# Second feed-forward stage with plain float32 matmuls over the whole array, and its inner layer on four 32-row strips

## The chip, the cores and the metric

One NeuronCore of a Trainium2 chip runs the whole kernel. TensorE multiplies, VectorE and ScalarE work on tiles in SBUF and read PSUM, GpSimd prepares some tiles in the first part, and the DMA queue that SyncE (SP) fills moves nearly all data. The metric is the device time of one execution in microseconds; the number to forecast is the median over the runs of the changed kernel.

## What is computed

A linear attention with decay (4 batches, 8 heads, 768 steps, heads of 48) gives x, 3072 tokens by 384. A soft mixture of 8 experts with 4 slots each follows, and then a feed-forward layer with a squared relu:

```
x = attention(r, k, v, w, u)                 # 3072 x 384
logits = x @ phi                             # 3072 x 32
d = softmax over tokens;  slot_input = d.T @ x          # 32 x 384
slot_out[e] = relu(slot_input[e] @ w1[e]) @ w2[e]       # 32 x 384
c = softmax over slots;   y = c @ slot_out   # 3072 x 384
h = relu(y @ w_in)                           # 3072 x 2048
out = (h * h) @ w_out                        # 3072 x 384
```

The last two lines are the second feed-forward stage, which the change is about.

## The kernel before

The kernel is written out per engine, with semaphores between them. Its first part (to about 360 us) is the attention, in eight rounds of loops over pairs of heads. Then come the transposes of x (L561), the logits (L584), the two softmaxes, the slots (L606), the experts' up projection (L624, in four 32-column strips of the array) and down projection (L647, `down`), and the transposes of c into `c_st` (L668, copied out by `copy_ct`).

The second stage never forms y. Since y @ w_in = c @ (slot_out @ w_in), the kernel first makes m = slot_out @ w_in, 32 x 2048. L680 writes it into one PSUM bank: row strip q of 32 partitions holds columns 512q to 512q + 511. So the inner layer is a contraction over 32 slots.

Before the change this stage runs on split operands. `F32R` (fp32r) is a data type of reduced precision for matmul operands; the trace has one record for such a matmul. A float32 tile is taken apart into a high part, rounded to F32R, and a low part, the rest. For m and c the parts lie one above the other on the 128 partitions: `c_rep` has four copies of c per token block, high, high, low, low (L873 and L1165), and `m_parts`, `spread` and L690 lay m out as `m_st`, 128 x 2048, so that one matmul over 128 rows adds the four cross products. For the outer layer `wo_high` and `wo_low` hold w_out in parts, made from `w_raw` in four quarters by ScalarE (`wo_split_high`, L295) and VectorE (`wo_split_low`, L1180).

The loop goes over 8 groups of three token blocks (384 tokens) and in each over 16 blocks fb of 128 inner features, 128 steps in all:

- TensorE, `hidden` (L698): one matmul, 384 tokens wide, two steps ahead, into one of two banks.
- ScalarE, `hidden_sq`: relu (L907), then square (L911).
- VectorE, `split`: `h_high` is the rounded copy (L1210), `h_low` the rest (L1212).
- TensorE, `product`: for each of the three token blocks high x high, high x low, low x high (L708, L709, L710) into that block's accumulator bank. Two sets of three accumulator banks alternate.
- ScalarE, `out_copy` (L918), in the second step of the next group: three accumulators into `o_sb`; SP stores them (L372).

SP starts w_out's transfers after the last transpose of c (L365), two quarters, and the other two as `w_raw` comes free (L368). The order of the work on each engine is the order of the code.

Of the kernel before, what the change touches and what calls it, by code (L numbers as in the profile page):

```python
# [22 lines left out]
F32 = mybir.dt.float32  # L23
# [7 lines left out]
def fused_kernel(nc, r, k, v, w, u, phi, w1, w2, w_in, w_out, out, debug=None):  # L31
# [23 lines left out]
    with ctx:  # L55
# [6 lines left out]
        def sem2(name):  # L62
# [11 lines left out]
        c_stack = ExitStack()  # L74

        c_rep = sb("c_rep", [P, NT, 4, SL], F32R, c=c_stack)
        c_stack.close()
        w_raw = sb("w_raw", [P, 2, 4, E_DIM])
# [41 lines left out]
        wo_high = sb("wo_high", [P, NF, E_DIM], F32R, c=over_w1)  # L120
        wo_low = sb("wo_low", [P, NF, E_DIM], F32R, c=over_w1)
# [9 lines left out]
        c_st = sb("c_st", [P, B * S], F32R, c=fin)  # L131
        m_st = sb("m_st", [P, DFF], F32R, c=fin)
        h_relu = [sb(f"h_relu{i}", [P, GT * P], c=fin) for i in range(2)]
        h_sq = [sb(f"h_sq{i}", [P, GT * P], c=fin) for i in range(2)]
        h_high = [sb(f"h_high{i}", [P, GT * P], F32R, c=fin) for i in range(2)]
        h_low = [sb(f"h_low{i}", [P, GT * P], F32R, c=fin) for i in range(2)]
# [12 lines left out]
        h_stack = ExitStack()  # L149
        h_sb = sb("h_sb", [P, FF], c=h_stack)  # L150
        h_stack.close()
        m_parts = sb("m_parts", [P, 2, 512], F32R)
        h_t = sb("h_t", [P, 2, FB, P])
        small = sb("small", [P, 256])
        spread = sb("spread", [P, 2, 4, SL], F32R)
# [47 lines left out]
        w_raw_loaded = [sem(f"w_raw_loaded{i}") for i in range(2)]  # L203
# [10 lines left out]
        m_full, m_high, m_low, m_rep = sem("m_full"), sem("m_high"), sem("m_low"), sem("m_rep")  # L214
        m_rep_copy = [sem(f"m_rep_copy_{e}") for e in ("act", "dve")]
        spread_set, c_high, c_low, ct_full = sem("spread_set"), sem("c_high"), sem("c_low"), sem("ct_full")
        ct_copy = [sem(f"ct_copy_{e}") for e in ("act", "dve")]
        wo_high_done, wo_low_done = sem("wo_high_done"), sem("wo_low_done")
        h_mm, relu_done, sq_done, high_done, low_done = (sem(n) for n in ("h_mm", "relu_done", "sq_done", "high_done",
                                                                          "low_done"))  # L220
        prod_mm, o_copy = sem("prod_mm"), sem("o_copy")
# [9 lines left out]
        acc_bank = (bank[0:3], bank[3:6])  # L231
        h_bank = bank[6:8]
        M_BANKS = (0, 3, 4, 5)
        WO_SPLIT_AT = (1, 4, 8)
# [57 lines left out]

        def wo_split_high(act, part):
            act.wait_ge(w_raw_loaded[part % 2], 16 * (part // 2 + 1))
            nc.scalar.activation(wo_high[:, 4 * part:4 * part + 4, :], w_raw[:, part % 2], ACT.Copy)\  # L295
                .then_inc(wo_high_done, 1)

        @block.sync
        def _(sp):
# [66 lines left out]
            for i in range(2):  # L366
                sp.wait_ge(wo_low_done, i + 1)
                sp.dma_start(w_raw[:, i], wo_v[:, 4 * (i + 2):4 * (i + 2) + 4]).then_inc(w_raw_loaded[i], 16)  # L368

            def store(g, par):  # L370
                sp.wait_ge(o_copy, GT * (g + 1))
                sp.dma_start(out_v[bass.ds(GT * g, GT)].rearrange("n p d -> p n d"), o_sb[par][:])\  # L372
                    .then_inc(stored[par], 16)

            with sp.Fori(0, GROUPS // 2) as gg:
                for par in range(2):
                    store(gg * 2 + par, par)
            for par in range(2):
                sp.wait_ge(stored[par], 16 * GROUPS // 2)

# [872 lines left out]
```

## Time and profile before

| | us |
|---|---|
| median of 3 runs | 645.51 |
| lowest, highest of these runs | 641.88, 651.84 |
| span of the profiled execution | 648.8 |
| busy in that span: TensorE, weight loads, VectorE, ScalarE, GpSimd | 519.0, 445.8, 436.0, 397.5, 64.7 |
| mean granted TensorE clock | 0.908 |

The profiled execution's own time is not given apart from these runs; its span of 648.8 us, from the first to the last instruction, lies between the second and the third of them. A granted clock of 1.00 is 2.4 GHz, 0.50 is 1.2 GHz. "PE" is TensorE's matmuls and "PEld" its weight loads; a matmul's record lasts until its last result is written, so records of matmuls that follow one another overlap. "w_hi", "w_lo" and "w_sb" are names that the profile gives to w2_hi, w2_lo and w1_sb.

### The profile page before, as it was taken

The numbers are of one execution on the slowest core, as the hardware profiler recorded it, in microseconds if no ns is written. First come the engines' busy times: TensorE is split into PE (matmuls) and PEld (weight loads), VectorE is DVE, ScalarE is ACT, GpSimd is POOL, SyncE is SP. The second block draws the span as 40 slices with busy tenths as digits, with TensorE's granted clock in tenths as the row PEclk, the third lists the DMA queues.
The fourth block names the chain that finished last, engine by engine and source line by source line (L and its number), as shares of the span: only waits on it lengthen the run. The fifth ranks groups of instructions, "written<-read, shape, count | busy, mean of one in ns | idle before, by whom it ended". The sixth has DMA issues, their size and how long they took to land.

```text
span 648.8 us, 20419 instructions
## 1 busy us (share of the span) xinstructions
PE 519.0 (80%) x8010; PEld 445.8 (69%) x8010; DVE 436.0 (67%) x968; ACT 397.5 (61%) x753; POOL 64.7 (10%) x79
## 2 busy tenths in 40 slices
PE   3756766877668668766686798699999999999996
PEld 2544655756457447564576434399999999999996
DVE  5668999898688688896797441465555555555553
ACT  3648686885576477865765313466566666656563
POOL 4011213112031031130310000000000000000000
PEclk9869898987698699886887899899999999999999
DMA  9995354362154143630057699311010101101010
GB/s 140 303 314 98 62 96 68 73 109 54 24 109 78 30 83 76 108 60 17 3 113 257 225 387 364 141 52 37 2 37 1 38 1 36 37 0 36 1 37 36
DMA packets 143325, 60.75 MB, mean 94 GB/s; under 512 B 126496, under 2 KB 139808, under 8 KB 142880
## 3 DMA queue, kind: packets, MB, share of 16 engines
q1 hardware_dynamic: 141264, 51.97, 33.9%
q10 hardware_dynamic: 2000, 7.86, 3.2%
q8 instruction: 51, 0.84, 0.6%
q14 instruction: 10, 0.08, 0.0%
HBM read 55.10 MB, written 4.72 MB: 92 GB/s over the span
## 4 chain that ended last, share of the span: by engine, by line
PE 63%; issue 13%; DVE 11%; ACT 10%; ACTq 1%; DVEq 1%; DMA 0%; SPq 0%
PE bank L708 11%; PE bank L710 10%; PE bank L709 10%; PE lbank L497 7%; ACT rkw L756 6%; PE tbank L449 4%; PE ybank L523 4%; PE bank L698 3%; DVE wprod L992 3%; DVE a_pack L1046 2%; PE tbank L459 2%; DVE rkw L1012 2%; PE bank L647 2%; PE bank L624 2%; PE bank L561 1%
## 5 line engine op out<-in xcount | busy, mean ns | idle before, releaser
L708 PE MATMUL bank<-wo_high,h_high 128*128 128x384 f32 x384 | 129.6, 337 | 1.8 <-DVE h_low L1212 1.6
L709 PE MATMUL bank<-wo_low,h_high 128*128 128x384 f32 x384 | 128.9, 336 | 0.0
L710 PE MATMUL bank<-wo_high,h_low 128*128 128x384 f32 x384 | 128.9, 336 | 0.0
L497 PE MATMUL lbank<-rhat,rkw 128*32 128x64 f32 x3456 | 81.5, 244 | 53.9 <-DVE a_pack L1046 36.8
L791 ACT ACTIVATE rhat<-rkw 48x384 f32<-48x384 f32 x160 | 85.0, 531 | 59.5 <-PE lbank L497 42.2
L497 PEld LDWEIGHTS lbank<-rhat,rkw 128*32 128x32 f32 x3456 | 69.9, 126 | 63.7 <-issue 61.9
L1210 DVE CAST h_high<-h_sq 128x384 fp32r<-128x384 f32 x128 | 46.0, 360 | 96.7 <-PE bank L710 87.9
L907 ACT ACTIVATE h_relu<-bank 128x384 f32<-128x384 f32 x128 | 62.9, 492 | 74.4 <-PE bank L698 74.1
L756 ACT ACTIVATE rkw<-tbank 128x384 f32<-128x384 f32 x96 | 74.4, 876 | 20.5 <-PE tbank L449 20.5
L449 PE MATMUL tbank<-ident,nat 128*128 128x128 f32 x288 | 62.7, 358 | 29.7 <-ACT rkw L756 16.7
L708 PEld LDWEIGHTS bank<-wo_high,h_high 128*128 128x128 f32 x384 | 72.6, 189 | 3.2 <-issue 2.8
L1212 DVE TENSOR_TENSOR h_low<-h_sq,h_high 128x384 fp32r<-128x384 f32 x128 | 71.5, 559 | 4.4
L449 PEld LDWEIGHTS tbank<-ident,nat 128*128 128x128 f32 x288 | 39.4, 175 | 50.7 <-ACT rkw L756 35.2
L709 PEld LDWEIGHTS bank<-wo_low,h_high 128*128 128x128 f32 x384 | 72.7, 189 | 0.0
L710 PEld LDWEIGHTS bank<-wo_high,h_low 128*128 128x128 f32 x384 | 72.5, 189 | 0.0
L911 ACT ACTIVATE h_sq<-h_relu 128x384 f32<-128x384 f32 x128 | 67.4, 527 | 4.1
L1012 DVE TENSOR_TENSOR rkw<-rkw,wprod 128x384 f32<-128x384 f32 x80 | 45.4, 571 | 15.3 <-PE lbank L497 14.8
L408 POOL COPY mov<-state 48x576 f32<-48x576 f32 x28 | 35.2, 1258 | 170.9 <-DVE state L1054 170.1
L1046 DVE COPY_PREDICATED a_pack<-masks,lbank 128x384 f32<-128x384 int32 x80 | 46.5, 581 | 0.2
L1001 DVE TENSOR_TENSOR rkw<-rkw,wprod 128x384 f32<-128x384 f32 x64 | 41.1, 642 | 5.0 <-ACT rhat L791 4.1
L698 PE MATMUL bank<-c_st,m_st 128*128 (+1 forms) x126 | 42.7, 339 | 0.3 <-ACT h_relu L907 0.3
L976 DVE COPY rhat<-rkw 48x384 f32<-48x384 f32 x32 | 16.5, 515 | 29.0 <-ACT rkw L756 28.4
(129 smaller groups left out, 639.2 us busy)
## 6 DMA issues: line engine op xcount, KB each, us to landing
w_sb<-in_moe_w_dram ACTq DMA_DIRECT2D x5, 1536.0 KB, 15.7
w_hi<-in_moe_w_dram SPq DMA_DIRECT2D x16, 384.0 KB, 8.1
nat<-in_r_dram SPq DMA_DIRECT2D x32, 144.0 KB, 3.2
nat<-in_k_dram SPq DMA_DIRECT2D x32, 144.0 KB, 3.8
nat<-in_w_dram SPq DMA_DIRECT2D x32, 144.0 KB, 3.9
mov<-in_v_dram SPq DMA_DIRECT2D x32, 144.0 KB, 3.3
v_tok<-in_v_dram SPq DMA_DIRECT2D x32, 144.0 KB, 3.3
w_sb<-in_moe_w_dram SPq DMA_DIRECT2D x3, 1536.0 KB, 7.4
```

What stands on the lines that cost most here:

```text
L449: last = nc.tensor.transpose(bank[:, i * P:(i + 1) * P], src, ident[:])
L497: last = nc.tensor.matmul(dst.rearrange("p (h t) -> p h t", h=2), kk[:, t0:t0 + SUB], rhat[s][:, :, tt:tt + SUB], start=True, stop=True)
L698: nc.tensor.matmul(h_bank[fb % 2][:, 0:GT * P], m_st[:, fb * P:(fb + 1) * P], c_st[:, bass.ds(g * (GT * P), GT * P)], start=True, stop=Tru ...
L708: nc.tensor.matmul(acc, hi, wo_high[:, fb, :], start=(fb == 0), stop=False)
L709: nc.tensor.matmul(acc, hi, wo_low[:, fb, :], start=False, stop=False)
L710: last = nc.tensor.matmul(acc, lo, wo_high[:, fb, :], start=False, stop=(fb == NF - 1))
L756: nc.scalar.activation(dst, src, ACT.Copy).then_inc(t_evac, 1)
L791: nc.scalar.activation(half_split(rhat[s][a:b, h, :], 1 << lv)[:, :, 1, :], half_split(rkw[s][a:b, 0, :], 1 << lv)[:, :, 1, :], ACT.Copy)\
L907: nc.scalar.activation(h_relu[fb % 2][:], h_bank[fb % 2][:, 0:GT * P], ACT.Relu).then_inc(relu_done, 1)
L911: nc.scalar.activation(h_sq[fb % 2][:], h_relu[fb % 2][:], ACT.Square).then_inc(sq_done, 1)
L1046: nc.vector.copy_predicated(a_pack[s][:].rearrange("p c h t -> p (c h) t"), mask, data)\
L1212: nc.vector.tensor_tensor(h_low[i][:], h_sq[i][:], h_high[i][:].bitcast(F32), ALU.subtract)\
```

## The change

The stage drops the split. `wo_sb` holds w_out as it is, `m_sb` is one copy of the PSUM bank with m, in its four row strips (128 x 512), and `c_rep` is four plain copies of c. The 128 blocks of the inner layer become 32 steps of four: step n is group g = n // 4 and k = n % 4, and its strip r (32 rows) gives feature block 4r + k. `hidden(n)` issues four matmuls over 32 rows each, into four banks. ScalarE does only the relu, VectorE multiplies the result by itself, into eight tiles. `product(n, r)` is three plain float32 matmuls of 128 rows, one per token block. The accumulators rotate through four banks, and at a group's start only the second and third matmul wait for an output copy. SP loads w_out in one transfer as soon as w1's place is free, behind the transfers of w2_hi, and the last group is stored block by block. The loops are written out.

The core of the diff:

```diff
-        wo_high = sb("wo_high", [P, NF, E_DIM], F32R, c=over_w1)
-        wo_low = sb("wo_low", [P, NF, E_DIM], F32R, c=over_w1)
+        wo_sb = sb("wo_sb", [P, NF, E_DIM], c=over_w1)
...
-        acc_bank = (bank[0:3], bank[3:6])
-        h_bank = bank[6:8]
+        h_bank = (bank[0], bank[1], bank[6], bank[7])
+        acc_bank = (bank[3], bank[4], bank[5], bank[2])
+        KS = NF // 4
+        STEPS = GROUPS * KS
+
+        def acc_of(n):
+            return acc_bank[n % 4]
...
-            sp.wait_ge(ct_full, CT_USES)
-            for i in range(2):
-                sp.dma_start(w_raw[:, i], wo_v[:, 4 * i:4 * i + 4]).then_inc(w_raw_loaded[i], 16)
...
+            sp.wait_ge(up_mm, 4)
+            sp.dma_start(wo_sb[:], wo_v).then_inc(wo_loaded, 16)
...
+            def hidden(n):
+
+                g, k = divmod(n, KS)
+                cols = slice(g * GT * P, (g + 1) * GT * P)
+                for r in range(4):
+                    if n:
+                        pe.wait_ge(relu_done, 4 * (n - 1) + r + 1)
+                    rows = slice(SL * r, SL * r + SL)
+                    nc.tensor.matmul(h_bank[r][:, 0:GT * P], m_sb[rows, k * P:(k + 1) * P], c_st[rows, cols],
+                                     start=True, stop=True).then_inc(h_mm, 1)
+
+            def product(n, r):
+                g, k = divmod(n, KS)
+                pe.wait_ge(sq_done, 4 * n + r + 1)
+                first, final = k == 0 and r == 0, k == KS - 1 and r == 3
                 for i in range(GT):
...
+                    at = GT * g + i
+                    if first and at >= 4:
+                        pe.wait_ge(o_copy, at - 3)
+                    last = nc.tensor.matmul(acc_of(at)[:, 0:E_DIM], h_sq[4 * (n % 2) + r][:, i * P:(i + 1) * P],
+                                            wo_sb[:, KS * r + k, :], start=first, stop=final)
+                    if i < GT - 1 and final:
+                        last.then_inc(acc_done, 1)
                 last.then_inc(prod_mm, 1)
...
+            pe.wait_ge(m_copied, 1)
+            hidden(0)
+            pe.wait_ge(wo_loaded, 16)
+            for n in range(STEPS):
+                for r in range(4):
+                    if r == 2 and n + 1 < STEPS:
+                        hidden(n + 1)
+                    product(n, r)
...
+            nc.scalar.activation(m_sb[:], bank[2][:, :], ACT.Copy).then_inc(m_copied, 1)
...
+            for n in range(STEPS):
+                g, k = divmod(n, KS)
+                for r in range(4):
+                    act.wait_ge(h_mm, 4 * n + r + 1)
+                    if n:
+                        act.wait_ge(sq_done, 4 * (n - 1) + r + 1)
+                    nc.scalar.activation(h_relu[r][:], h_bank[r][:, 0:GT * P], ACT.Relu).then_inc(relu_done, 1)
+                if k == 0 and g:
+                    for i in range(GT):
+                        out_copy(GT * (g - 1) + i)
...
             for q in range(2):
-                nc.vector.tensor_tensor(c_part(2 + q), cc[:], c_part(q).bitcast(F32), ALU.subtract).then_inc(c_low, 1)
...
+                nc.vector.tensor_copy(c_part(2 + q), cc[:]).then_inc(c_spread, 1)
...
+            for n in range(STEPS):
+                for r in range(4):
+                    dve.wait_ge(relu_done, 4 * n + r + 1)
+                    if n >= 2:
+                        dve.wait_ge(prod_mm, 4 * (n - 2) + r + 1)
+                    nc.vector.tensor_tensor(h_sq[4 * (n % 2) + r][:], h_relu[r][:], h_relu[r][:], ALU.mult)\
+                        .then_inc(sq_done, 1)
```

On TensorE, from m (L680) to the first products, the order before is:

```order
L680 MATMUL bank<-w_in_sb,slot_ot 32x512 x11
L690 MATMUL bank<-m_parts,spread 128x512 [waits m_low,m_high,spread_set]
L690 MATMUL bank<-m_parts,spread 128x512 x7
L730 MATMUL bank<-c_st,m_st 128x384 [waits m_rep_copy_act]
L730 MATMUL bank<-c_st,m_st 128x384
L698 MATMUL bank<-c_st,m_st 128x384 [waits relu_done]
L708 MATMUL bank<-wo_high,h_high 128x384 [waits low_done,high_done,wo_low_done]
L709 MATMUL bank<-wo_low,h_high 128x384
L710 MATMUL bank<-wo_high,h_low 128x384
```

and now, where L659, L671 and L682 are the lines of m, `hidden` and `product`:

```order
L659 MATMUL bank<-w_in_sb,slot_ot 32x512 x11
L671 MATMUL bank<-c_st,m_sb 128x384 [waits m_copied]
L671 MATMUL bank<-c_st,m_sb 128x384 x3
L682 MATMUL bank<-wo_sb,h_sq 128x384 [waits sq_done,wo_loaded]
L682 MATMUL bank<-wo_sb,h_sq 128x384 x2
L682 MATMUL bank<-wo_sb,h_sq 128x384 [waits sq_done]
L682 MATMUL bank<-wo_sb,h_sq 128x384 x2
L671 MATMUL bank<-c_st,m_sb 128x384 [waits relu_done] x4
```

The eight matmuls that lay m out are gone, one block of the inner layer per nine products has become four strips per twelve, and the first product waits for the load of all of w_out.

On TensorE at the start of the third group now, with its waits:

```order
L671 MATMUL bank<-c_st,m_sb 128x384 [waits relu_done] x4
L682 MATMUL bank<-wo_sb,h_sq 128x384 [waits sq_done]
L682 MATMUL bank<-wo_sb,h_sq 128x384 x2
L682 MATMUL bank<-wo_sb,h_sq 128x384 [waits sq_done]
L682 MATMUL bank<-wo_sb,h_sq 128x384 x2
L682 MATMUL bank<-wo_sb,h_sq 128x384 [waits sq_done]
L682 MATMUL bank<-wo_sb,h_sq 128x384 [waits o_copy] x2
```

The next step's strips stand two product blocks ahead of its first product, and of a group's first three matmuls the second and third wait for a copy.

## Rows read from the trace of the kernel before

**Rows 1.** the page's chain that ended last, by line

```profile
PE bank L708 11%; PE bank L710 10%; PE bank L709 10%; PE lbank L497 7%; ACT rkw L756 6%; PE tbank L449 4%; PE ybank L523 4%; PE bank L698 3%; DVE wprod L992 3%; DVE a_pack L1046 2%; PE tbank L459 2%; DVE rkw L1012 2%; PE bank L647 2%; PE bank L624 2%; PE bank L561 1%
```

**Rows 2.** stretches by busy us (instructions) of each engine, clock, DMA share, GB/s

```profile
413.40:419.61 6.21, 2.23 (x12) 0.96 (x12) 4.62 (x7) 5.84 (x9) 0.00 (x0) 0.75 0.06 11
419.61:643.96 224.35, 224.15 (x1277) 222.82 (x1277) 121.19 (x257) 138.54 (x276) 0.00 (x0) 0.99 0.07 26
643.96:648.80 4.84, 0.00 (x0) 0.00 (x0) 0.00 (x0) 1.25 (x3) 0.00 (x0) 0.98 0.33 122
453.28:481.04 27.76, 27.76 (x161) 27.75 (x161) 14.70 (x32) 17.34 (x35) 0.00 (x0) 1.00 0.06 23
416.60:423.40 6.80, 4.92 (x15) 4.11 (x14) 5.76 (x9) 4.49 (x9) 0.00 (x0) 0.50 0.42 121
```

**Rows 3.** one group by lines: count, busy us, mean ns, idle before

```profile
L710 PE MATMUL bank<-wo_high,h_low 128*128 128x384 f32 x48 | 16.0, 334 | 0.0
...
L1212 DVE TENSOR_TENSOR h_low<-h_sq,h_high 128x384 fp32r<-128x384 f32 x16 | 8.9, 559 | 0.6
...
L907 ACT ACTIVATE h_relu<-bank 128x384 f32<-128x384 f32 x16 | 7.9, 492 | 9.4 <-PE bank L698 9.4
```

**Rows 4.** line L602, its weight loads in time, and that stretch

```profile
L602 PE MATMUL bank<-dd,ones x4: 844/844/1006, 370.3 to 372.4; 128*128 128x384 f32 x4
...
371.10 0.33 PEld L602 LDWEIGHTS bank<-dd,ones 128*128 128x128 f32 x1 [0.30 <-issue]
371.74 0.33 PEld L602 LDWEIGHTS bank<-dd,ones 128*128 128x128 f32 x1 [0.31 <-issue]
...
370.40:373.20 2.80, 2.80 (x8) 1.11 (x11) 1.24 (x3) 0.84 (x1) 0.00 (x0) 0.50 1.07 376
```

**Rows 5.** in order of time after m, and line L690 (durations ns min/median/max)

```profile
413.40 0.60 ACT L895 ACTIVATE m_parts<-bank 128x512 fp32r<-128x512 f32 x1 [3.88 <-PE bank L680]
...
414.87 0.75 PE L690 MATMUL bank<-m_parts,spread 32*128 32x512 f32 x8 [1.53 <-DVE m_parts L1196]
...
L690 PE MATMUL bank<-m_parts,spread x8: 391/427/496, 414.9 to 415.2; 32*128 32x512 f32 x8
```

**Rows 6.** float32 on four column strips, L647

```profile
403.59 5.37 PE L647 MATMUL bank<-w_hi,h_t 128*32 128x384 f32 x64
...
L647 PE MATMUL bank<-w_hi,h_t x64: 486/486/510, 403.6 to 408.5; 128*32 128x384 f32 x64
```

**Rows 7.** column strips, whole array, strips again, in time; lines and clock

```profile
272.30 0.68 PE L497 MATMUL lbank<-rhat,ku 128*32 128x64 f32 x35
272.90 1.60 PE L505 MATMUL ybank<-ones 128*128 128x128 f32 x12
274.44 0.77 PE L497 MATMUL lbank<-rhat,rkw 128*32 128x64 f32 x40
...
272.90 0.71 PE L505 MATMUL ybank<-ones 128*128 128x128 f32 x4
...
L505 PE MATMUL ybank<-ones x160: 275/275/582, 22.6 to 339.0; 128*128 128x128 f32 x160
...
L497 PE MATMUL lbank<-rhat,rkw x3456: 216/219/316, 27.0 to 338.0; 128*32 128x64 f32 x192
...
272.50:275.00 2.50, 2.50 (x87) 2.29 (x79) 2.47 (x7) 2.40 (x5) 0.00 (x0) 1.00 1.20 185
```

**Rows 8.** the DMA engines ahead of the products

```profile
404.00:410.00 6.00, 5.39 (x67) 2.07 (x59) 0.39 (x1) 0.49 (x1) 0.00 (x0) 1.00 0.98 334
410.00:416.00 6.00, 3.65 (x34) 1.02 (x32) 1.39 (x5) 2.37 (x3) 0.00 (x0) 1.00 0.01 2
```

**Rows 9.** VectorE's relu h_sb, behind c_low and spread, and line L624

```profile
386.78 0.68 DVE L1174 TENSOR_SCALAR h_sb<-bank 128x512 f32<-128x512 f32 x1
...
L624 PE MATMUL bank<-w_sb,slot_t x96: 592/592/617, 380.3 to 390.2; 128*32 128x512 f32 x96
```

**Rows 10.** the last output copies, after the last product

```profile
643.99 1.25 ACT L918 ACTIVATE o_sb<-bank 128x384 f32<-128x384 f32 x3 [3.63 <-PE bank L710]
```

More of the change, by code:

```diff
@@ L130, in fused_kernel @@
         fin = ExitStack()
[L131 to L136, printed above, removed]
+        c_st = sb("c_st", [P, B * S], c=fin)
+        m_sb = sb("m_sb", [P, DFF // 4], c=fin)
+        h_relu = [sb(f"h_relu{i}", [P, GT * P], c=fin) for i in range(4)]
+        h_sq = [sb(f"h_sq{i}", [P, GT * P], c=fin) for i in range(8)]
         o_sb = [sb(f"o_sb{i}", [P, GT, E_DIM], c=fin) for i in range(2)]
@@ L213, in fused_kernel @@
         down_mm, so_copy, so_turned, so_ready = sem("down_mm"), sem("so_copy"), sem("so_turned"), sem("so_ready")
[L214 to L216 removed]
+        m_full, m_copied = sem("m_full"), sem("m_copied")
+        c_spread, ct_full = sem("c_spread"), sem("ct_full")
         ct_copy = [sem(f"ct_copy_{e}") for e in ("act", "dve")]
[L218 to L221, printed above, removed]
+        h_mm, relu_done, sq_done = sem("h_mm"), sem("relu_done"), sem("sq_done")
+        prod_mm, acc_done, o_copy = sem("prod_mm"), sem("acc_done"), sem("o_copy")
         stored = [sem("stored0"), sem("stored1")]
@@ L660, in _ @@
             turn_slots(0)
-            pe.wait_ge(c_high, 2)
-            pe.wait_ge(c_low, 2)
+            pe.wait_ge(c_spread, 4)
             for n in range(CT_USES):
@@ L682, in _ @@
             last.then_inc(m_full, 1)
-            pe.wait_ge(spread_set, 8)
-            pe.wait_ge(m_high, 1)
-            pe.wait_ge(m_low, 1)
-            for n in range(4):
-                rows = slice(SL * n, SL * n + SL)
-                for x in range(2):
-                    last = nc.tensor.matmul(bank[M_BANKS[n]][:, :], spread[rows, x].rearrange("p q j -> p (q j)"),
-                                            m_parts[rows, x, :], start=(x == 0), stop=(x == 1))
-                last.then_inc(m_rep, 1)
@@ L713, in group @@
-            def group(g, par, lead=True, wait_acc=True, first=False):
-                for fb in range(NF):
-                    if fb < NF - 2:
-                        if first and fb % 4 == 2:
-                            n = (fb + 2) // 4
-                            pe.wait_ge(m_rep_copy[n % 2], n // 2 + 1)
-                        hidden(g, fb + 2)
-                    elif lead:
-                        hidden(g + 1, fb + 2 - NF)
-                    if fb == 0 and wait_acc:
-                        pe.wait_ge(o_copy, GT * (g - 1))
-                    if first and fb % 4 == 0:
-                        pe.wait_ge(wo_low_done, fb // 4 + 1)
-                    product(g, par, fb)
@@ L728, in _ @@
-            pe.wait_ge(m_rep_copy[0], 1)
-            for fb in range(2):
-                nc.tensor.matmul(h_bank[fb][:, 0:GT * P], m_st[:, fb * P:(fb + 1) * P], c_st[:, 0:GT * P],
-                                 start=True, stop=True).then_inc(h_mm, 1)
-            group(0, 0, wait_acc=False, first=True)
-            group(1, 1, wait_acc=False)
-            with pe.Fori(1, GROUPS // 2 - 1) as gg:
-                group(gg * 2, 0)
-                group(gg * 2 + 1, 1)
-            group(GROUPS - 2, 0)
@@ L913, in out_copy @@
-            def out_copy(g, par, first=False):
-                act.wait_ge(prod_mm, NF * (g + 1))
-                if not first:
-                    act.wait_ge(stored[par], (g - par) * 8)
-                for i in range(GT):
-                    nc.scalar.activation(o_sb[par][:, i, :], acc_bank[par][i][:, 0:E_DIM], ACT.Copy)\
-                        .then_inc(o_copy, 1)
-            def group(g, par, before=True, first=False):
-                for fb in range(NF):
-                    hidden_sq(g, fb, fresh=(not before and fb < 2))
-                    if not before and fb in WO_SPLIT_AT:
-                        wo_split_high(act, WO_SPLIT_AT.index(fb) + 1)
-                    if fb == 1 and before:
-                        out_copy(g - 1, 1 - par, first)
```

134 lines of the change are left out of this document (27 added, 107 removed).

## The prediction

> **What bounds the kernel now.** I read the chain that ended last first. It puts 63% of the span on TensorE, and its three largest lines are the three products of the second feed-forward stage, L708 to L710 [rows 1]. Then the stretches by stage [rows 2]: that stage runs from 419.61 to 643.96 us, 224.35 us or 35% of the span, and TensorE is busy for 224.15 of it. Then one group of it by lines [rows 3]: 144 product records and 16 hidden-layer records fill 27.76 us, so 0.1735 us from one matmul to the next. A record lasts 0.334 us, about twice that, because each overlaps its neighbour: it is the spacing that counts, not the duration. VectorE is busy for 14.70 and ScalarE for 17.34 of the 27.76 us. So this stage is bound by TensorE's columns, and what matters is how many passes of 384 columns the changed stage makes and at what spacing.
>
> All my sums are made inside the profiled execution, whose span is 648.8 us. The runs shown are 641.88, 645.51 and 651.84 us; only the last is long enough to contain that span, with 3.0 us around it. I work out a difference of spans and add it to the median, 645.5. About 2% (13 us) is what a measurement of this kernel can tell from no change.
>
> **The change part by part.**
>
> *Products, the large term.* Removed: 1152 split products of 384 columns at 0.1735 us, 199.9 us. Added: 384 matmuls (32 steps of 4 strips of 3 blocks) in plain float32. What does one cost? The kernel has plain float32 matmuls already. L602 issues two, of 128x128 against 384 columns, exactly the shape of the new ones, and the trace has four records [rows 4]: one such matmul is two records. They run while the granted clock is 0.50 (1.2 GHz), and the weight loads of the last two start 0.64 us apart (371.10, 371.74). At 2.4 GHz that is 0.32 us for a record, two cycles per column, where a split matmul at that clock takes 0.1735 for one record of as many columns. There are two such records to a matmul, so a block costs four passes of 384 columns where it cost three.
> At the high clock there is a small addition to each record. Bounds: in four column strips L647 puts 64 records into 5.37 us [rows 6]; less the last one's 0.486 that is 4.88 over 15 steps of four, 0.325 each. No addition at all, 0.320, is the lowest. The split products have 0.0135 over the ideal 0.160; the same on each 0.320 gives 0.3335, the highest. The row nearest in shape is L505, a plain float32 128x128 matmul of 128 columns at the clock of 1.00: 12 records in 1.60 us, 4 in 0.71 [rows 7], so 8 spacings in 0.89, 0.111 each, where 0.32 us for 384 columns would be 0.107 for 128. That is 0.004 to 0.005 on top, weight load of 128 columns included. Both point to 0.325, and I take that. 384 x 2 x 0.325 = **249.6 us** (245.8 to 256.1). A weight load under each record is no term of its own: L505 hides one under 0.111 us.
>
> *Hidden layer on four strips.* Removed: 128 matmuls at 0.1735, 22.2 us (two of them before 419.61). Added: 32 rounds of four 32-row matmuls, 31 of them inside the stage. In m_rep's matmuls (L690) the kernel has four row strips of 32: eight records of 512 columns lie within 0.75 us [rows 5], where one after the other they would need 8 x 512/384 x 0.16 = 1.7 us. So strips do overlap, even though the two matmuls of a strip stand next to each other in the program. Two float32 records per strip are then 0.645 us for all four. In L690 the last record, of 0.39 us, starts 0.75 - 0.39 = 0.36 us after the first, 0.15 more than 512 columns take (0.213): I add 0.15. Crossing between strips and the whole array also costs: the last L497 record starts at 272.98 - 0.22 = 272.76, L505 at 272.90; that is 0.14 where fours of L497 follow each other at (0.68 - 0.22) / 8.5 = 0.055, 0.09 more. L505's first spacing is 0.71 - 0.275 - 2 x 0.111 = 0.21, 0.10 more than its others. Back, L497 starts at 274.44, 0.21 after the last L505 (272.90 + 1.60 - 0.275 = 274.23), again 0.10 more [rows 7]. Together 0.29 per round trip. So a round is 0.645 + 0.15 + 0.29 = 1.08 us and 31 of them **33.5 us**. Bounds: 0.65 (no crossing, no stagger), 20.2 us; or strips that don't overlap at all, which is a rival below.
> By the Trainium skill, TensorEngine Tiling (Array Packing), section Key Properties, changing the tiling mode drains the TensorE. The trace shows less than that: by its recorded ends L505 begins 0.08 us before L497 is over. If each of the 62 crossings waited for the recorded end (0.486 - 0.325 = 0.16 us, [rows 6], instead of some 0.095), the sum would be 4 us higher, 706 us.
>
> *Clock.* After the idle stretch ahead of the products, TensorE stood at 1.2 GHz from 416.6 to 423.4 us [rows 2], 3.8 us of it under products: 1.9 us lost. The new start has idle waits of the same kind, so I keep **1.9 us** (0 to 3.4).
>
> *The stage.* 249.6 + 33.5 + 1.9 + 0.2 for the last record's tail = 285.2 against 224.35.
>
> *Start.* Now: m_full, split into m_parts, spread (L690), m_st, first hidden block, relu, square, and on VectorE a wo_low ahead of m_st's second part and h_high: 413.40 to 419.61, 6.21 us [rows 2]. New: one copy of m (0.60, as that of m_parts, [rows 5]), strips from 414.03, first strip done after 0.15 + 0.32 + 0.49 = 0.96 at 415.0, relu 0.49, multiply 0.56 (h_low's subtraction, two operands of the same size, [rows 3]), some 0.05 of waiting: first product at 416.1. **Minus 3.5 us.** It also needs the whole w_out. SP now issues it in one transfer right behind the 16 of w2_hi, not in quarters from 403.7 on. The DMA engines are full until 410 (0.98 busy, 334 GB/s) and then idle (2 GB/s) [rows 8], and half of w_out (1.57 MB) is already in that traffic. The other half takes 1.57 MB at 334 GB/s = 4.7 us: it lands near 414.7. Hidden, with 1.4 us to spare; if all of it came after 410, products would start at 419.4, 3.3 us later. It has nothing behind it on SP until the first store. The work taken from VectorE and ScalarE earlier (c_low, spread, the wait of c_low for c_high) ends when VectorE turns to h_sb at 386.78, and TensorE needs that only behind L624, whose last record starts at 390.2 [rows 9]: nothing gained.
>
> *Per step beside TensorE.* A step is 24 x 0.325 + 1.08 = 8.9 us. ScalarE has four relus (2.0 us), VectorE four multiplies (2.2 us). Behind the strips of the next step stand two product blocks of 3 x 0.65 = 1.95 us each, 3.9 us, and the first multiply is due 1.1 us after its strip. The wait for an output copy at a group's start covers itself: the freed block was finished three matmuls (1.95 us) earlier, the copy takes 0.49. Both hidden; uncovered they would cost 7 to 8 group starts x 0.5 = 4 us.
>
> *End.* Three copies after the last product (1.25 us, [rows 10]) become one (0.49): **minus 0.8 us**. The last store is a third in size; I keep the 3.6 us behind the copies (bound: 1.2 us less).
>
> Sum: 416.1 + 285.2 = 701.3, + 4.84 - 0.76 = 705.4 us of span, 56.6 more than 648.8. 645.5 + 56.6 = **702.1 us**, 8.8% slower.
>
> **The rivals.**
> A (other side): whole-array float32 records run at the pace of the split ones, 0.174 us, at the high clock. Then products are 768 x 0.174 = 133.6 us and the span 589, the time 586 us. It decides from 0.251 us per record (235.4 us from 413.40 to the end, less 42.4 of new fixed terms, over 768); with 0.268 it would be 2% slower. For: fewer instructions, and no row has this exact shape at 2.4 GHz. Against: L602 and L505 both show two cycles per column in every record.
> B: 32-row strips in float32 don't overlap. Each round is 4 x 0.65 + 0.44 = 3.04, 31 x 1.96 = 61 us more, 763 us. For: L690 is split, not float32. Against: L690 overlaps with its pair of matmuls per strip, L647 overlaps in float32 on column strips.
> C: weight loads for float32 are laid bare, 0.10 us a record (what L505's first spacing shows over its others): 77 us more, 779 us. Against: L505's later spacings, L602's 0.64.
> D: the products start late or wait once per group (w_out, copies): 2 to 6 us, inside my range.
>
> **How the numbers follow.** Forecast 0.90, A 0.03, B 0.04, C 0.03. The forecast's own range: low, 20.2 instead of 33.5 for the strips and 3.8 less in records, 685; high, 6.5 more for the products and 3.3 for w_out, 712. Both extremes at once are unlikely, but the runs before spread by some 4 to 6 us either way: 688 to 717. That holds about 8 in 10 with the rivals left out. Faster by over 2%: only A, 0.02. Within 2%: A in part, 0.01. Slower by over 2%: 0.97.
>
> **What would show it.** Right: two records per product matmul, weight loads hidden, spacing 0.325; the stage some 285 us long; steps of 8.9 us, of which the strips take about 1.1; first product near 416; VectorE and ScalarE under a third busy there, clock 1.00. Wrong: record spacing below 0.27 (A) or above 0.4 (C), rounds of strips near 3 us (B), product matmuls that wait for sq_done or o_copy, a first product after 418.

## The result, and the profile after

The changed kernel takes 704.43 us (median of 4 runs, 697.38 to 705.90) against 646.83 us for the kernel before (4 runs, 641.88 to 651.84): a ratio of 1.088 with a 95% interval of 1.080 to 1.096. It is slower by nearly 9%, and the forecast was 702.1 us. All ratios leave out runs that were over 1.5% above the fastest of the same kernel. The profiled execution has a span of 704.0 us, 55.2 more than before; I had worked out 56.6.

The page's table of engines, the lines of the new stage and its clock answer to [rows 1, 3]:

```profile
PE 581.1 (83%) x7746; PEld 382.1 (54%) x7746; DVE 370.7 (53%) x825; ACT 317.6 (45%) x619; POOL 65.3 (9%) x79
...
PEclk9989978669985799868889999999999999999999
...
L682 PE MATMUL bank<-wo_sb,h_sq 128*128 128x384 f32 x768 | 256.2, 490 | 1.2 <-DVE h_sq L1127 1.2
L682 PEld LDWEIGHTS bank<-wo_sb,h_sq 128*128 128x128 f32 x768 | 143.3, 190 | 112.0 <-issue 16.9
L1127 DVE TENSOR_TENSOR h_sq<-h_relu 128x384 f32<-128x384 f32 x128 | 62.9, 554 | 214.2 <-ACT h_relu L869 214.2
L869 ACT ACTIVATE h_relu<-bank 128x384 f32<-128x384 f32 x128 | 52.4, 496 | 199.7 <-PE bank L671 199.7
...
L671 PE MATMUL bank<-c_st,m_sb 32*128 32x384 f32 x256 | 29.7, 533 | 0.7 <-ACT m_sb L851 0.7
```

Each of the 384 product matmuls is two records (x768), each of the 128 strip matmuls too (x256). TensorE is all but never idle before them (1.2 us), while VectorE and ScalarE sit idle some 200 us: the stage is bound by TensorE alone, more so than before. The slices of the stage stand at clock 9, which means 90% or more.

By stretches, in the columns of [rows 2] (copy of m to first product; the loop; from the last product's end; one step of the loop):

```profile
417.66:420.48 2.82, 0.93 (x8) 0.34 (x9) 0.70 (x2) 1.82 (x5) 0.00 (x0) 1.00 0.22 78
420.48:701.10 280.62, 280.62 (x1016) 152.93 (x1016) 62.17 (x127) 62.50 (x149) 0.00 (x0) 1.00 0.04 15
701.10:704.00 2.90, 0.00 (x1) 0.00 (x0) 0.00 (x0) 0.49 (x1) 0.00 (x0) 1.00 0.57 203
566.10:574.89 8.79, 8.79 (x36) 4.79 (x32) 1.96 (x4) 1.64 (x4) 0.00 (x0) 1.00 0.01 2
```

Start 2.82 us (6.21 before), loop 280.62 (224.35), end 2.90 (4.84). From the copy of m to the end of the span that is 286.3 us instead of 235.4: 50.9 us of the 55.2 arise in the changed stage. The other 4.3 lie ahead of it: the copy of m starts at 417.66 instead of 413.40. There the code is the same but for the copies of c and the time at which w_out's load is issued, and its place in time varies between executions. In the profiles below, all of nearly the same code up to there, the copy starts at anything from 411.6 to 418.7. The new load isn't the cause of the shift: 3.9 of the 4.3 us were there at the first up projection (384.24 instead of 380.30), and the load is issued at 402.8.

One step of the loop on TensorE, and what ScalarE and VectorE do beside it:

```profile
566.10 8.01 PE L682 MATMUL bank<-wo_sb,h_sq 128*128 128x384 f32 x24
566.18 1.64 ACT L869 ACTIVATE h_relu<-bank 128x384 f32<-128x384 f32 x4 [4.22 <-PE bank L671]
566.71 1.96 DVE L1127 TENSOR_TENSOR h_sq<-h_relu 128x384 f32<-128x384 f32 x4 [6.83 <-ACT h_relu L869]
...
574.03 0.93 PE L671 MATMUL bank<-c_st,m_sb 32*128 32x384 f32 x8
...
574.89 1.56 PE L682 MATMUL bank<-wo_sb,h_sq 128*128 128x384 f32 x4
```

A column gives the start, the next the time to the end of the last record. 24 product records (12 matmuls: the last two blocks of one step and the first two of the next) begin at 566.10, the strips at 574.03, the next products at 574.89. A step is 574.89 - 566.10 = 8.79 us. The products' 24 records end at 574.11, and the last one lasts 0.486: so from the first start to the last it is 7.52 us, over 23 spacings. The first of these is 0.43 (1.56 us for four records at 574.89, less 0.486 and two spacings), the others 0.3225 each. VectorE's last multiply ends at 568.67, 2.6 us after the products start. The next step's first product is the 13th record, at about 570.1, so ScalarE and VectorE have at least 1.4 us to spare.

### The profile page after: what moved, and what is told of

Its sections match the earlier page's. It is cut to its first block, busy times and chain, and to the rows that moved or that the text cites. A ratio compares the mean times of both kernels' runs of the same rounds, so it can differ in the third digit from the quotient of the medians.

```text
span 704.0 us, 19073 instructions
## 1 busy us (share of the span) xinstructions
PE 581.1 (83%) x7746; PEld 382.1 (54%) x7746; DVE 370.7 (53%) x825; ACT 317.6 (45%) x619; POOL 65.3 (9%) x79
## 4 chain that ended last, share of the span: by engine, by line
PE 63%; issue 12%; ACT 10%; DVE 10%; SPq 2%; DMA 2%; ACTq 1%; DVEq 1%
PE bank L682 36%; PE lbank L477 6%; ACT rkw L713 6%; PE tbank L429 4%; PE bank L671 4%; PE ybank L503 4%; DVE wprod L930 2%; DVE a_pack L984 2%; PE lbank L453 2%; SPq L345 2%; DVE rkw L950 2%; PE tbank L439 1%; DMA w_hi<-in_moe_w_dram 1%; DVE rkw L939 1%; PE bank L541 1%
## 5 line engine op out<-in xcount | busy, mean ns | idle before, releaser
L682 PE MATMUL bank<-wo_sb,h_sq 128*128 128x384 f32 x768 | 256.2, 490 | 1.2 <-DVE h_sq L1127 1.2
L682 PEld LDWEIGHTS bank<-wo_sb,h_sq 128*128 128x128 f32 x768 | 143.3, 190 | 112.0 <-issue 16.9
L1127 DVE TENSOR_TENSOR h_sq<-h_relu 128x384 f32<-128x384 f32 x128 | 62.9, 554 | 214.2 <-ACT h_relu L869 214.2
L429 PEld LDWEIGHTS tbank<-ident,nat 128*128 128x128 f32 x288 | 40.2, 178 | 50.9 <-ACT rkw L713 35.0
L503 PE MATMUL ybank<-mov,stat 112*64 112x48 f32 (+1 forms) x768 | 32.1, 245 | 4.4 <-issue 4.4
L503 PEld LDWEIGHTS ybank<-mov,stat 112*64 112x64 f32 (+1 forms) x768 | 29.7, 158 | 7.1 <-issue 6.5
L398 POOL COPY stat<-rkw 48x384 f32<-48x384 f32 x32 | 23.0, 720 | 100.2 <-DVE rkw L939 97.3
L671 PE MATMUL bank<-c_st,m_sb 32*128 32x384 f32 x256 | 29.7, 533 | 0.7 <-ACT m_sb L851 0.7
L930 DVE TENSOR_TENSOR wprod<-wprod 128x192 f32<-128x192 f32 (+4 forms) x80 | 27.2, 340 | 0.0
L439 PE MATMUL tbank<-ident,rkw 112*128 112x112 f32 x96 | 16.7, 311 | 12.0 <-issue 9.3
L992 DVE TENSOR_TENSOR_SCAN state<-w_scan,kv 112x576 f32<-112x576 f32 x16 | 21.7, 1354 | 4.4 <-ACT kv L728 4.4
```

Of the source, the lines that this page charges most:

```text
L429: last = nc.tensor.transpose(bank[:, i * P:(i + 1) * P], src, ident[:])
L503: last = nc.tensor.matmul(ybank[C * par:C * par + C, o:o + D], stat[s][h][0:rows, c, :], mov[s][h][0:rows, c, :], start=True, stop=True)
L671: nc.tensor.matmul(h_bank[r][:, 0:GT * P], m_sb[rows, k * P:(k + 1) * P], c_st[rows, cols], start=True, stop=True).then_inc(h_mm, 1)
L682: last = nc.tensor.matmul(acc_of(at)[:, 0:E_DIM], h_sq[4 * (n % 2) + r][:, i * P:(i + 1) * P], wo_sb[:, KS * r + k, :], start=first, stop= ...
L1127: nc.vector.tensor_tensor(h_sq[4 * (n % 2) + r][:], h_relu[r][:], h_relu[r][:], ALU.mult)\
```

## The experiments

Since the unchanged part shifts by several microseconds from one execution to the next, I compare, next to the times, three stretches of each profile, cut as above: start, loop, end.

| kernel | start | loop | end | from copy of m | time, us |
|---|---|---|---|---|---|
| before | 6.21 | 224.35 | 4.84 | 235.4 | 646.8 |
| changed | 2.82 | 280.62 | 2.90 | 286.3 | 704.4 |
| plain products only | 4.73 | 271.86 | 4.93 | 281.5 | 695.0, ratio 1.069 (1.058 to 1.080) |
| strips only | 4.77 | 240.98 | 2.94 | 248.7 | 664.1, ratio 1.017 (1.005 to 1.029) |
| no rounds | 2.82 | 249.61 | 2.91 | 255.3 | 672.3 |
| double rounds | 3.46 | 300.62 | 2.91 | 307.0 | 722.6 |
| rounds cut in two | 2.82 | 314.20 | 2.86 | 319.9 | 740.4 |
| late load | 2.82 | 282.32 | 2.85 | 288.0 | 707.4 |
| bfloat16 parts | 6.21 | 214.49 | 4.85 | 225.6 | 643.2, ratio 0.984 (0.969 to 1.000) |
| combined | 5.29 | 212.18 | 3.03 | 220.5 | 639.8, ratio 0.981 (0.971 to 0.991) |

Ratios are to runs of the kernel before that were made beside each kernel. Their median was 652.1 us beside the plain products, the strips and the bfloat16 parts, and 652.7 us beside the combined kernel, not the 646.8 us of the result. Times are medians of all runs of a kernel; one without a ratio, from the third row on, is a single run. Each kernel has one profile.

**One part alone: plain float32 products.** The inner layer stays one split matmul per block.

```diff
                 for i in range(GT):
                     acc = acc_bank[par][i][:, 0:E_DIM]
-                    hi, lo = (a[fb % 2][:, i * P:(i + 1) * P] for a in (h_high, h_low))
-                    nc.tensor.matmul(acc, hi, wo_high[:, fb, :], start=(fb == 0), stop=False)
-                    nc.tensor.matmul(acc, hi, wo_low[:, fb, :], start=False, stop=False)
-                    last = nc.tensor.matmul(acc, lo, wo_high[:, fb, :], start=False, stop=(fb == NF - 1))
+                    last = nc.tensor.matmul(acc, h_sq[fb % 2][:, i * P:(i + 1) * P], wo_sb[:, fb, :],
+                                            start=(fb == 0), stop=(fb == NF - 1))
```

> The kernel before with only the outer layer changed to plain float32 products (w_out whole, in one transfer); the inner layer stays one split matmul over the whole array per block. Theory (a float32 record of 384 columns is 0.3225 us, a round of strips 1.055 us): the loop holds 768 x 0.3225 + 126 x 0.1735 = 269.6 us against 280.6 of the changed kernel, the start is some 1.7 us longer and the end 0.8 us, so 704.4 - 11.0 + 2.5 = 696 us. Rival (the strips are what made it slow, by waits or crossings that the sum put elsewhere): 670 us or less. Rival (changing between float32 and split matmuls costs like a crossing, 0.4 us per step of 128): 745 us.

Measured 695.0 us. The loop, and the pace in it:

```profile
411.58:416.31 4.73, 2.37 (x12) 1.12 (x12) 1.98 (x3) 2.84 (x6) 0.00 (x0) 0.81 0.06 23
416.31:688.17 271.86, 271.86 (x894) 168.46 (x893) 0.00 (x0) 122.44 (x275) 0.00 (x0) 0.99 0.04 16
```

```profile
560.01 2.10 PE L696 MATMUL bank<-wo_sb,h_sq 128*128 128x384 f32 x6
561.65 0.63 PE L688 MATMUL bank<-c_st,m_st 128*128 x1
562.12 2.10 PE L696 MATMUL bank<-wo_sb,h_sq 128*128 128x384 f32 x6
```

Steps stand 2.11 us apart (560.01, 562.12): six float32 records at 0.3225 and 0.17 for the split one between them, with no price for the change of type. 271.86 us of loop is 2.3 above the 269.6 expected. The clock explains that: a stretch at 1.2 GHz reached 5 us into the products (granted clock 0.51 from 416.31 to 421.40 us) and cost 2.5. The plain products alone bring 46.1 of the 50.9 us from the copy of m: they are the change's cost, and both rivals fall. That the time came within 1 us of the 696 expected is in part luck, since the kernel before was 5.3 us slower beside this run than in the result.

**The other part alone: strips.** The changed kernel with split products, their parts made by ScalarE and VectorE, and w_out loaded in four parts as before.

```diff
                 for i in range(GT):
...
-                    last = nc.tensor.matmul(acc_of(at)[:, 0:E_DIM], h_sq[4 * (n % 2) + r][:, i * P:(i + 1) * P],
-                                            wo_sb[:, KS * r + k, :], start=first, stop=final)
+                    acc = acc_of(at)[:, 0:E_DIM]
+                    hi, lo = (a[r][:, i * P:(i + 1) * P] for a in (h_high, h_low))
+                    nc.tensor.matmul(acc, hi, wo_high[:, 4 * k + r, :], start=first, stop=False)
+                    nc.tensor.matmul(acc, hi, wo_low[:, 4 * k + r, :], start=False, stop=False)
+                    last = nc.tensor.matmul(acc, lo, wo_high[:, 4 * k + r, :], start=False, stop=final)
```

> The changed kernel with only its inner layer kept (four row strips in plain float32, 32 steps), its products in split form as before, their parts made by VectorE and ScalarE. Theory: the loop is 1152 x 0.1735 + 31 x 1.055 = 232.6 us against 224.35 before, the start about 2 us shorter, the end 1 us, no time at the low clock 2 us: 646.8 + 3 = 650 us. Rival (strips save what they were meant to, 4 x 0.1735 become 0.65 with crossings hidden): 643 us. Rival (ScalarE's square and VectorE's split no longer keep up with four strips at once): above 660 us, with products waiting for low_done.

Measured 664.1 us, a miss: 14 us above the theory, ratio 1.017 where I had said 1.005. About 5 of the 14 us are in the kernel before too (652.1 instead of 646.8). The loop is 8.4 us longer than the 232.6 I gave it, and the waits in it (who waited for whom: us in total, times, longest) name one part:

```profile
417.41:422.18 4.77, 0.93 (x8) 0.34 (x9) 2.73 (x4) 4.67 (x9) 0.00 (x0) 0.86 0.00 0
422.18:663.16 240.98, 237.80 (x1400) 210.59 (x1400) 120.02 (x257) 129.82 (x277) 0.00 (x0) 0.99 0.07 25
```

```profile
PEld bank L698 <- ACT o_sb L886: 5.4, 7, 0.8
```

At seven group starts TensorE waits for the output copies, 0.77 us each, 5.4 in all. In the changed kernel it never does. The rows of the first such start here:

```profile
452.85 0.33 PE L700 MATMUL bank<-wo_high,h_low 128*128 128x384 f32 x1
...
454.24 0.52 ACT L896 ACTIVATE h_sq<-h_relu 128x384 f32<-128x384 f32 x1
454.67 1.24 ACT L886 ACTIVATE o_sb<-bank 128x384 f32<-128x384 f32 x3
...
455.20 0.44 PE L698 MATMUL bank<-wo_high,h_high 128*128 128x384 f32 x1 [0.45 <-ACT o_sb L886]
```

The group's first accumulator had its last record at 452.85, so it was complete at 453.2, but ScalarE began to copy it only at 454.67, right behind the last square. Four relus and four squares take it 3.8 us per step here, and the copies stand behind them in its order. In the changed kernel it has the relus alone (1.64 us), and there all 24 copies wait for a product. So the wait comes from ScalarE's squares and from where the copies stand. That is read from the trace; no run moved the copies. Another 2.7 us are the low clock at the start (granted clock 0.51 from 422.18 to 427.80 us). 5.4 + 2.7 = 8.1 of 8.4 us. The first rival falls (strips save nothing: a round is 1.06 us here too). The second is half right: no product waits for low_done in the loop, but ScalarE's squares do hold the products up, by way of the copies. The start was 4.77 us where I expected some 4.2: the first product waited for the first part of w_out's low half. From the copy of m to the end, the four kernels of this two by two give 46 us for the products, 13 for the strips, and 51, not 59, for both. Of these 8.5 us less, 5.4 are the copies' waits, which the changed kernel doesn't have, and 3.3 are the clock (1.9 us lost before, 2.5 with plain products, 2.7 with strips, none in the changed kernel).

**Rounds left out.** This kernel leaves the inner layer, relu and square out after the first step and multiplies the first four tiles again, so products no longer wait for squares.

```diff
                 for r in range(4):
-                    if r == 2 and n + 1 < STEPS:
-                        hidden(n + 1)
                     product(n, r)
```

> The changed kernel without the inner layer after the first step: products use the first four tiles again, so relu and squares are left out too. Theory: 31 rounds x 1.055 us go, and from the copy of m to the end it takes 286.3 - 32.7 = 253.6 us, with float32 records 0.3225 us apart throughout; the time is near 704 - 33 = 671 us. Rival (crossings cost nothing, a round is worth only its records, 0.65 us): 266 us from the copy, 684 in all. Rival (products also wait on relu or squares somewhere): below 248 us from the copy.

```profile
415.16:417.98 2.82, 0.93 (x9) 0.35 (x9) 0.71 (x2) 1.82 (x5) 0.00 (x0) 1.00 0.09 34
417.98:667.59 249.61, 249.61 (x768) 146.82 (x768) 1.25 (x3) 11.68 (x25) 0.00 (x0) 0.99 0.05 17
```

The span is 670.5 us. The loop of 249.61 us is 768 x 0.3225 = 247.7, the last record's 0.2 and 1.7 for 3.4 us at the low clock just behind the start (granted clock 0.54 from 417.98 to 421.70 us). Without that clock the rounds weigh 280.62 - 247.9 = 32.7 us, 31 x 1.055. The 1.055 was itself taken from the changed kernel's loop; what this run shows is that the 32.7 us go with the rounds, to 0.1 us, and that the first rival (0.65 us a round) and the second (products that wait) fall; 255.3 us from the copy of m lies 1.7 above the 253.6 expected, by the clock.

**Each round twice.**

```diff
-                for r in range(4):
-                    if n:
+                for x in range(2):
+                    for r in range(4):
+                        if n and not x:
...
+                        if x:
+                            last.then_inc(h_mm, 1)
```

> The changed kernel with each round of four strips issued twice, back to back, into the same banks. Theory (a round is 0.645 us of records and 0.41 us of crossing and bare weight loads, paid once per round trip): 32 x 0.645 = 20.6 us more, span 725 us. Rival (the 0.41 us belongs to every round of 128-column weights in 32-row strips): 32 x 1.055 = 33.8 us more, 738 us. Rival (strips of the second round overlap the first): less than 10 us more.

```profile
417.27:717.89 300.62, 300.62 (x1264) 165.72 (x1264) 62.17 (x127) 62.49 (x149) 0.00 (x0) 1.00 0.04 14
```

```profile
562.91 1.57 PE L672 MATMUL bank<-c_st,m_sb 32*128 32x384 f32 x16
564.41 8.01 PE L685 MATMUL bank<-wo_sb,h_sq 128*128 128x384 f32 x24
```

The loop grows by 300.62 - 280.62 = 20.0 us, 0.645 for each of its 31 rounds: 16 strip records in 1.57 us instead of 8 in 0.93. A second round costs its two records and nothing else. So 0.645 + 0.41 is the right split, the 0.41 us is paid per round trip, and both rivals fall.

**Each round cut in two.**

```diff
-                    if r == 2 and n + 1 < STEPS:
-                        hidden(n + 1)
+                    if r in (1, 2) and n + 1 < STEPS:
+                        hidden(n + 1, range(2 * r - 2, 2 * r))
```

> The changed kernel with each round of four strips cut in two: strips 0 and 1 after a step's first product block, strips 2 and 3 after its second. Same matmuls, twice the crossings, two strips side by side instead of four. Theory (a round costs 0.645 us of records and 0.41 us of crossing, whatever the number of strips in it): the loop grows by 31 x 1.055 = 32.7 us to 313 us, some 737 us in all. Rival (strips share the array's time, two cost half of four): 31 x 0.41 = 12.7 us more, 717 us. Rival (the crossing hides behind products when fewer strips wait): no change.

```profile
421.54:735.74 314.20, 314.20 (x1016) 159.79 (x1016) 64.97 (x127) 65.81 (x149) 0.00 (x0) 0.99 0.04 14
```

```profile
562.87 0.92 PE L671 MATMUL bank<-c_st,m_sb 32*128 32x384 f32 x4
563.71 2.20 PE L682 MATMUL bank<-wo_sb,h_sq 128*128 128x384 f32 x6
565.84 0.91 PE L671 MATMUL bank<-c_st,m_sb 32*128 32x384 f32 x4
```

The loop is 314.20 us. Less 1.7 for the clock that fell behind the start (0.62 from 421.54 to 426.00 us) it is 312.5, 31.9 more than the changed kernel's; 32.7 were expected. Two strips take as long as four (4 records in 0.91, 8 in 0.93), and each further round trip costs 0.4 us. Both rivals fall.

**The load of w_out late.**

```diff
-            sp.wait_ge(up_mm, 4)
+            sp.wait_ge(ct_full, CT_USES)
             sp.dma_start(wo_sb[:], wo_v).then_inc(wo_loaded, 16)
```

> The changed kernel with w_out's one transfer issued behind the last transpose of c, as before the change, instead of behind TensorE's last up projection. Theory (the DMA engines are full until it has landed, so they set the landing and not the time of issue, some 4 us later): start and total as in the changed kernel, 2.8 us from the copy of m to the first product, 286 us from that copy to the end. Rival (the early issue is what hides the load): first product 3 to 5 us later, 290 us from the copy. It also shows whether the experts' down projection then still waits for w2_hi (0.8 us in the changed kernel): by the theory it waits as long, since the queue works in order; by the rival that w_out's transfer takes bandwidth from w2_hi's, it does not.

In both kernels the rows are the issue by SP, the time to landing, and TensorE's longest wait for w2_hi (w_hi), first the changed kernel's:

```profile
402.83 0.95 SPq L348 DMA_DIRECT2D wo_sb<-in_moe_w_out_dram  x1
```

```profile
DMA to landing us min/median/max: 17.3/17.3/17.3
```

```profile
  PEld bank L627: 0.8, 1
```

and with the late load:

```profile
407.91 0.37 SPq L348 DMA_DIRECT2D wo_sb<-in_moe_w_out_dram  x1
```

```profile
DMA to landing us min/median/max: 11.9/11.9/11.9
```

```profile
PEld bank L627 <- DMA w_hi<-in_moe_w_dram: 0.3, 1, 0.3
```

The early transfer is issued at 402.8 and lands after 17.3 us, at 420.1; the late one at 407.9, and lands after 11.9, at 419.8. The DMA engines set the landing, not the time of issue (in the changed kernel their busy share is 1.00 from 384 to 420 us, at 365 GB/s), and from the copy of m to the first product it is 2.82 us in both. The wait for w2_hi is 0.8 us with the early load and 0.3 with the late one; I had expected it to stay. The other profiles leave open whether the early transfer takes bandwidth from w2_hi: with it the wait was 0.8, 0, 0 and 2.3 us (plain products, no rounds, cut in two, double rounds), with a late one 0, 0.6, 0.2 and 0.2 (before, strips, bfloat16 parts, combined). It may be worth up to 2 us, all of it ahead of the stage. The loop is 1.7 us longer here by the clock: it fell behind the start (0.63 from 420.43 to 425.00 us), and did not in the changed kernel's profile.

**Bfloat16 parts.** The kernel before, with the high and low parts of w_out and of h squared in bfloat16.

```diff
-        wo_high = sb("wo_high", [P, NF, E_DIM], F32R, c=over_w1)
-        wo_low = sb("wo_low", [P, NF, E_DIM], F32R, c=over_w1)
+        wo_high = sb("wo_high", [P, NF, E_DIM], BF16, c=over_w1)
+        wo_low = sb("wo_low", [P, NF, E_DIM], BF16, c=over_w1)
...
-        h_high = [sb(f"h_high{i}", [P, GT * P], F32R, c=fin) for i in range(2)]
-        h_low = [sb(f"h_low{i}", [P, GT * P], F32R, c=fin) for i in range(2)]
+        h_high = [sb(f"h_high{i}", [P, GT * P], BF16, c=fin) for i in range(2)]
+        h_low = [sb(f"h_low{i}", [P, GT * P], BF16, c=fin) for i in range(2)]
```

> The kernel before with the high and low parts of w_out and of the squared hidden layer in bfloat16 instead of fp32r; the inner layer stays fp32r. It measures what the 0.0135 us over 384 columns in each split matmul is. Theory (it belongs to operands of four bytes at one cycle per column): spacing 0.1625 us, 1152 x 0.011 = 12.7 us less, 634 us. Rival (it belongs to every whole-array matmul with a new 128-column weight load, or to accumulation in one bank): no change, 646 us.

```profile
424.86:639.35 214.49, 213.88 (x1277) 126.80 (x1277) 121.21 (x257) 137.65 (x276) 0.00 (x0) 0.99 0.08 27
```

```profile
521.33 0.33 PE L709 MATMUL bank<-wo_high,h_high 128*128 128x384 bf16 x1
521.49 0.33 PE L710 MATMUL bank<-wo_low,h_high 128*128 128x384 bf16 x1
521.65 0.33 PE L711 MATMUL bank<-wo_high,h_low 128*128 128x384 bf16 x1
521.68 0.47 PE L699 MATMUL bank<-c_st,m_st 128*128 x1
522.00 0.34 PE L709 MATMUL bank<-wo_high,h_high 128*128 128x384 bf16 x1
```

The loop is 214.49 us, 9.9 less. A step of ten matmuls (521.33 and so on) shows bfloat16 matmuls 0.16 to 0.165 apart, where fp32r ones stood 0.1735 apart. The time is 0.984 of before with an interval that touches 1, so by itself it shows no gain. The loop, which is free of the other part's scatter, does: it gained the 12.7 us of the theory less 2.8. The fp32r matmul of the inner layer accounts for 2.4 of these: a step is 1.655 us and not 9 x 0.1625 + 0.1735 = 1.636.

**What the runs point to, combined.** The kernel before with bfloat16 for all split parts of the stage (also m and c), w_out's first quarter split while ScalarE and VectorE wait for m, and the last group copied and stored block by block as in the change.

```diff
-        c_st = sb("c_st", [P, B * S], F32R, c=fin)
-        m_st = sb("m_st", [P, DFF], F32R, c=fin)
+        c_st = sb("c_st", [P, B * S], BF16, c=fin)
+        m_st = sb("m_st", [P, DFF], BF16, c=fin)
...
             slots_out(1)
+            wo_split_high(act, 0)
             act.wait_ge(m_full, 1)
...
+            for i in range(GT):
+                sp.wait_ge(o_copy, GT * (GROUPS - 1) + i + 1)
+                sp.dma_start(out_v[GT * (GROUPS - 1) + i], o_sb[1][:, i, :]).then_inc(stored[1], 16)
```

> The kernel before with what the runs so far point to: high and low parts of h squared, w_out, m and c in bfloat16 (0.1625 us instead of 0.1735 per matmul of 384 columns), w_out's first quarter split while ScalarE and VectorE wait for m, and the last group copied and stored block by block, as in the changed kernel. Theory: 1280 matmuls x 0.011 = 14 us less, start 1 us, end 2 us less: from the copy of m to the end 235.4 - 17 = 218.5 us, the time some 630 us, 2.6% below before. Rival (only the products' parts gain, the inner layer's matmul between them pays a change of type): 221 us from the copy. Rival (the gain of the bfloat16 parts was that run's luck): 232 us from the copy.

```profile
417.50:422.79 5.29, 1.62 (x11) 0.41 (x12) 3.05 (x6) 3.73 (x8) 0.00 (x0) 0.81 0.47 149
422.79:634.97 212.18, 211.29 (x1277) 124.71 (x1277) 121.35 (x257) 139.16 (x278) 0.00 (x0) 0.99 0.07 24
```

```profile
520.45 0.33 PE L718 MATMUL bank<-wo_high,h_low 128*128 128x384 bf16 x1
520.61 0.33 PE L706 MATMUL bank<-c_st,m_st 128*128 x1
520.77 0.33 PE L716 MATMUL bank<-wo_high,h_high 128*128 128x384 bf16 x1
520.94 0.33 PE L717 MATMUL bank<-wo_low,h_high 128*128 128x384 bf16 x1
```

639.8 us, 0.981 of before (0.971 to 0.991): faster than both kernels, by less than the 2.6% expected. From the copy of m it is 220.5 us, 14.9 less than before and 2.0 above the expectation. By that number alone the first rival (221 us) is nearer, but its reason is not there: ten matmuls follow each other at 0.1625 us throughout. The loop of 212.18 us is 1278 x 0.1625 = 207.7, the last record's 0.2, 2.3 for the low clock (0.50 from 422.79 to 427.60 us), and 0.9 in which TensorE is idle (212.18 less 211.29). The remaining 1.1 us are not accounted for. The runs compare time alone; what bfloat16 parts do to the error of the result was not compared.

## Why the prediction was right

*The large term.* "Two records of 0.325 for one matmul": in the changed kernel they stand 0.3225 apart, so 247.7 us instead of the 249.6 of the sum. The run without rounds has the same pace (32 records in 10.48 us). So of the 0.005 that I added after L505 and L647, half was there; why those rows have more, no run shows. The main step, four passes for three, is what made the kernel slower, and the run with plain products alone shows it: 46 of 51 us. Rivals A and C, pace of the split matmuls or bare weight loads, are gone by the same row. One reading in this step is not secured: that the pace before, 0.1735 us, was that of TensorE's columns. In [rows 2] its weight loads are as busy as its matmuls (27.75 of 27.76 us in one group), which the last section takes up. The forecast took the 0.1735 us as measured and doesn't hang on it.

*The rounds.* 33.5 us were predicted and 32.7 measured, of which the runs with no, double and halved rounds confirm both parts: 0.645 of records, 0.41 per round trip. The pieces I had added (0.15, 0.09, 0.10, 0.10) come to 0.44. Rival B, strips in float32 that don't overlap, is gone: four take as long as two. By the Trainium skill, TensorEngine Tiling (Array Packing), section Key Properties, changing the tiling mode drains the TensorE. Here the strips begin at 574.03, before the products' recorded end at 574.11, by the same 0.08 us as in [rows 7], so the switch doesn't wait for the recorded end. That end is modelled, and not observed as the last result's, so the trace doesn't tell whether the array was drained by then. How the 0.41 us divides between the switch, the bare first weight loads and the stagger of the strips was not measured apart.

*The clock.* This term was right in kind and wrong as a constant: 1.9 us predicted, none in the changed kernel's profile. With the same start to 0.01 us, the clock stayed at 2.4 GHz in the changed kernel and fell to 1.2 GHz for 3.4 us behind the start in three of its variants, which cost each 1.7 us. With one profile each, no run tells whether that goes with the single execution or with the kernel.

*The start.* 2.70 us predicted, 2.82 measured. The load of w_out was to have 1.4 us to spare. It had some 0.2: it landed at 420.1, and the first square, for which the first product waited to 420.48, was done at 420.35. So that it stayed hidden was close. The time of issue did not matter, as the late load shows. The prediction named a first product after 418 as a sign of being wrong; it came at 420.48, but only because the copy of m came 4.3 us later.

*The end.* The mis-sized term: 4.08 us predicted, 2.90 measured. I kept the 3.6 us behind the copies, although the last store is a third in size. Its landing took 1.9 us instead of the 3.0 before:

```profile
L357 SPq DMA_DIRECT2D out_dram<-o_sb x3: 332/350/351, 700.4 to 701.7; - x3
...
DMA to landing us min/median/max: 1.9/1.9/1.9
```

*The sum.* The stage was predicted to take 292.0 us from the copy of m and took 286.3: 1.9 too much for the products, 0.8 for the rounds, 1.9 for the clock, 1.2 for the end, 0.1 too little for the start. The time, within 2.3 us of the forecast, hit it more closely than the stage did, and that is luck: the unchanged part took 4.3 us more in the profiled execution. That part varies by 7 us between the profiles, and so an error of 5.7 us in the stage could not be seen in the time.

## What to carry to other kernels

Before choosing between plain float32 and split operands, count passes: plain float32 made two records of two cycles per column, four passes, against three for the split with one cross term left out. The engines that did the splitting had time to spare, so that what the change saved there was worth nothing. And where row strips share the array with whole-array matmuls, put as much strip work as the banks allow between two crossings, since a round trip cost about the same, 0.38 to 0.41 us, for two strip matmuls as for four and eight. And work that was free on an idle engine is not free in another order: with four squares in a row ahead of the output copies, ScalarE held TensorE up at every group start.

## What was not expected of the hardware

- A split matmul of 384 columns takes 0.1735 us in fp32r and 0.1625 in bfloat16 (384 columns at 2.4 GHz are 0.160); a plain float32 record, twice as long, adds only 0.0025. What fp32r adds doesn't come from accumulating in one bank, which all three do. The weight load is a rival that no run excludes. The rows are from the kernel before and from the one with bfloat16 parts:

```profile
L709 PEld LDWEIGHTS bank<-wo_low,h_high x384: 187/188/338, 419.7 to 643.3; 128*128 128x128 f32 x192
...
L710 PEld LDWEIGHTS bank<-wo_low,h_high x384: 95/98/152, 424.9 to 638.7; 128*128 128x128 bf16 x192
```

  In fp32r a weight load is recorded with 0.188 us, longer than the columns take, and weight loads fill 222.82 of the loop's 224.35 us [rows 2]. In bfloat16 they last 0.098 us and fill 126.80 of 214.49. In plain float32 they last 0.190, but under records 0.3225 apart. So the kernel before may be bound by its weight loads as much as by its columns.
- Of four starts that were equal to 0.01 us (2.82 us from the copy of m to the first product), one kept TensorE at 2.4 GHz, and in three it fell to 1.2 GHz for 3.4 us behind them.
- A change of type between whole-array matmuls (float32 and fp32r, 126 times) costs nothing that shows at 0.01 us; between bfloat16 and fp32r a step is some 0.02 us longer, which may be the longer weight load of that one fp32r matmul just as well.
